# Two heads on the two halves of the TensorE array: the k-v and q products of a fused attention, MLP and gating kernel

## The chip, the cores and the metric

The kernel runs on one NeuronCore of a Trainium2 chip. The metric is the time of one execution on the device, in microseconds (us). The kernel before takes 1369.3 us, the median of 3 runs (1369.15 to 1370.15).

## The reference

Batch 8, 8 heads, sequence 576, head size 64, all float32. Three stages follow each other. The first is a linear attention with a norm over each head:

```python
kv = np.einsum('bhsd,bhse->bhde', k, v)          # per head 64 x 64
out = np.einsum('bhsd,bhde->bhse', q, kv)        # per head 576 x 64
rms = np.sqrt(np.mean(out * out, axis=-1, keepdims=True) + 1e-06)
attn = out / rms * g_norm
```

The second stage takes the result as x (8 x 576 x 512), adds a low-rank product along the sequence (u = x + (x^T U V)^T) and an MLP with 2048 hidden units (u + relu(u w_ch1) w_ch2). The third is a gated MLP: h = gelu(x w_in), its second half normalised and mixed along the sequence by w_sg (576 x 576), multiplied with the first half, then w_out and the residual. Only the first stage's two products, kv and out, are touched by the change.

## The kernel before, in words

**Stages.** In the first 60 us the attention of batch 0 is computed. Then the up products of the MLP (x w_ch1, by a scheme of seven products on blocks) run for batch 0 to 7, one tile per batch; into the steps of tile t the attention of batch t + 1 is interleaved. After some 515 us the down products follow (to about 945 us) and then the gated MLP. Large products are done as three products of a high and a low part (`product`, L1366 to L1368).

**Attention.** Two heads make a pair; HP = 4 pairs a batch, 32 in all. k_raw, v_raw and q_raw hold a pair's inputs, rows on the partitions in NJ = 5 groups (the last of 64 rows, padded with zeros). For one pair m:
- `q_transposed` (transposes at L1371) puts q of both heads, 64 + 64 columns, on the partitions: qT is 128 x 5 x 128, the first head on partitions 0 to 63, the second on 64 to 127. ScalarE copies it out of PSUM (`q_copy` L656, `q_copy_tail` L660).
- `k_v` (L1387) multiplies k^T and v of both heads at once: 5 accumulating products of 128 x 128 by 128 x 128. Only the two 64 x 64 blocks on the diagonal are wanted. `kv_copy` (L666 on ScalarE in the loop, L1067 on VectorE in the first rounds) copies these two into kv, whose other two blocks were set to zero once, by a memset on GpSimd (POOL, L594).
- `attention` (L1395, L1397) multiplies qT (stationary, 128 x 128 for each of the 5 groups) with the block-diagonal kv (moving, 128 x 128). Four groups fill one PSUM bank (BX = 6), the fifth goes to the next (BY = 7).
- ScalarE copies the result into y, in two activations (`attn_copy`, L671 for the bank of four groups, L673 for the fifth), then squares it (L677). VectorE sums the squares (L968), ScalarE takes the root (L681), VectorE inverts and multiplies (L972, L975), then high and low parts are made (L685, L979), and `low_rank` (L1403) and `u_transposed` (L1371, L1414) finish the pair. The result leaves by x_raw (L697).

All these products are plain float32. Each appears in the trace as two passes, and a pass is one LDWEIGHTS (engine row PEld) and one MATMUL (engine row PE). So the 5 products of k_v or of attention are 10 passes.

**What orders the work.** Each engine's program is written out by hand, and semaphores tie them. In the up stage a tile has STEPS = 56 steps of 6 products. `attention_step` hangs the pair's pieces behind certain steps of a period of 12: attention behind step 0, q_transposed and k_v of the next pair behind step QK = 2, low_rank behind step 8, u_transposed behind step 11. Before q_transposed PE waits for s_o, the counter of y copies, since the transposes go into the banks that attention filled. Before attention it waits for s_uev, the copy of the former pair's result. s_out counts finished parts of attention, s_zero the memsets at the start. VectorE's sums of the up products (`added`, L1047 to L1061) free the PSUM banks for PE's next steps.

Of the kernel before, what the change touches and what calls it, by code (L numbers as in the profile page):

```python
# [7 lines left out]
ACT = mybir.ActivationFunctionType  # L8
AX = mybir.AxisListType

P = 128
B, H, S, HD = 8, 8, 576, 64
# [5 lines left out]
NJ = 5  # L18
JM = 4
# [6 lines left out]
HP = H // 2  # L26
# [53 lines left out]
def build(nc, q, k, v, g_norm, U, V, w_ch1, w_ch2, w_in, g_ln, w_sg, b_sg, w_out, out):  # L80
# [35 lines left out]
    k_raw = at("k_raw", [P, NJ, 2, HD], F32)  # L116
    v_raw = at("v_raw", [P, 2, NJ, HD], F32)
    q_raw = at("q_raw", [P, NJ, 2, HD], F32)
    qT = at("qT", [P, NJ, P], F32)
    part = at("part", [P, P], F32)  # L120
    kv = at("kv", [P, P], F32)
    y = at("y", [P, NJ, P], F32)
# [19 lines left out]
    k_raw = [k_raw] + [at(f"k_raw{i}", [P, NJ, 2, HD], F32) for i in range(1, HP)]  # L142
# [71 lines left out]
    with ExitStack() as ctx:  # L214
# [7 lines left out]
        s_zero = sem("tails_zeroed")  # L222
# [357 lines left out]
        @block.gpsimd  # L580
        def _(pool):

            nc.gpsimd.memset(identF[:], 0.0).then_inc(s_zero, 1)
            for i in range(HP):
                nc.gpsimd.memset(k_raw[i][:, JM, :, :], 0.0).then_inc(s_zero, 1)
                nc.gpsimd.memset(v_raw[i][:, :, JM, :], 0.0).then_inc(s_zero, 1)
                nc.gpsimd.memset(q_raw[i][:, JM, :, :], 0.0).then_inc(s_zero, 1)
            nc.gpsimd.memset(eps_col[:], EPS).then_inc(s_zero, 1)
            nc.gpsimd.memset(half_neg[:], -0.5).then_inc(s_zero, 1)
            nc.gpsimd.memset(U_raw[:, JM, :], 0.0).then_inc(s_zero, 1)  # L590
            pool.wait_ge(s_zero, 3 * HP + 4)
            nc.gpsimd.affine_select(out=identF[:], in_=identF[:], compare_op=ALU.not_equal, fill=1.0, base=0,
                                    pattern=[[-1, P]], channel_multiplier=1).then_inc(s_idF, 1)
            nc.gpsimd.memset(kv[:], 0.0).then_inc(s_zero, 1)  # L594
            nc.gpsimd.memset(V_aug[:, S:].bitcast(F32), 0.0).then_inc(s_zero, 1)
            pool.dma_start(U_raw[:, 0:JM, :], U[0:SM, :].rearrange("(p j) r -> p j r", j=JM)).then_inc(s_small, 16)
            pool.dma_start(U_raw[0:ST, JM, :], U[SM:S, :]).then_inc(s_small, 16)
            for n in range(4):
                pool.dma_start(V_raw[R * n:R * (n + 1), :], V[:, :]).then_inc(s_small, 16)

            def load_w1(part, pairs):

                for slot, kh, fh in ((0, 0, 0), (4, 0, 1), (3, 1, 0), (6, 1, 1)):
                    for c in range(2):
                        at_ = slice(0, 2) if part == 0 else slice(pairs.start - 2, pairs.stop - 2)
                        pool.dma_start(w1_raw[min(part, 1)][:, at_, 1, slot, c * P:(c + 1) * P],
                                       w_ch1[(2 * kh + c) * P:(2 * kh + c + 1) * P,
                                             (NPAIR * fh + pairs.start) * P:(NPAIR * fh + pairs.stop) * P].rearrange("p (a m) -> p a m", m=P)
                                       ).then_inc(s_w1[part], 16)

            pool.wait_ge(s_kv, 1)
            load_w1(0, slice(0, 2))
            pool.wait_ge(s_kv, 3)
            load_w1(1, slice(2, 4))
            pool.wait_ge(s_kv, HP)
            load_w1(2, slice(4, NPAIR))
            for g in range(2, NG):
                pool.wait_ge(s_p, 2 * NI * (g - 2) + 4)
                w1_sums(pool, nc.gpsimd, g)


            def x2_low(p, par):
                n = (NJ * P, S)[par]
                pool.wait_ge(s_x2hi, 2 * p + par + 1)
                nc.gpsimd.tensor_tensor(x2_lo[par][:, :, 0:n], x2_raw[par][:, :, 0:n], x2_hi[par][:, :, 0:n].bitcast(F32),
                                        ALU.subtract).then_inc(s_x2lo, 1)

            def inverse_std(p, par):
                for j in range(VB[par], VB[par + 1]):
                    pool.wait_ge(s_var, NCP * p + j + 1)  # L630
                    nc.gpsimd.tensor_tensor(rs[:, j % 3, :], ve[:, j % 3, :], half_neg[:], ALU.pow).then_inc(s_rs, 1)

            pool.wait_ge(s_pb, NSL * (NTILE - 1) + 24)
            nc.gpsimd.memset(ws_raw[:, 0:JM, SM:SM + ST], 0.0).then_inc(s_wst, 1)
            nc.gpsimd.memset(ws_raw[:, 0:JM, SM + 2 * ST:], 0.0).then_inc(s_wst, 1)
            nc.gpsimd.memset(ws_raw[:, JM, :], 0.0).then_inc(s_wst, 1)
            inverse_std(0, 0)
            x2_low(0, 1)
            with pool.Fori(0, B // 2 - 1) as i:
                inverse_std(i, 1)  # L640
                x2_low(i + 1, 0)
                inverse_std(i + 1, 0)
                x2_low(i + 1, 1)
            inverse_std(B // 2 - 1, 1)
# [3 lines left out]
        def _(act):  # L648
            def bank(n, a, b):
                return ps[:, n, a:b]  # L650

            def q_copy(m, bx, first=False):
                act.wait_ge(s_qt, 2 * m + 1)
                if not first:
                    act.wait_ge(s_out, 2 * m)
                nc.scalar.activation(qT[:, 0:JM, :].rearrange("p j m -> p (j m)"), ps[:, bx], ACT.Copy).then_inc(s_qsb, 1)  # L656

            def q_copy_tail(m, by):
# [8 lines left out]

            def attn_copy(m, bx, by, y=y):

                act.wait_ge(s_out, 2 * m + 1)  # L670
                nc.scalar.activation(y[:, 0:JM, :].rearrange("p j m -> p (j m)"), ps[:, bx], ACT.Copy).then_inc(s_o, 1)  # L671
                act.wait_ge(s_out, 2 * m + 2)
                nc.scalar.activation(y[:, JM, :], bank(by, 0, P), ACT.Copy).then_inc(s_o, 1)  # L673

            def squares(m, sq, y=y):
                act.wait_ge(s_o, 2 * (m + 1))
                nc.scalar.activation(sq[:], y[:], ACT.Square).then_inc(s_sq, 1)  # L677

            def std(m):
# [54 lines left out]
            for n in range(2):  # L734
                act.dma_start(gcol[HD * n:HD * (n + 1), :], g_norm.rearrange("(p o) -> p o", o=1)).then_inc(s_g, 16)

            act.wait_ge(s_zero, 3 * HP + 6)
            q_copy(0, 0, first=True)
            q_copy_tail(0, 1)
            for m in range(HP):  # L740
# [224 lines left out]
        def _(dve):  # L965
# [100 lines left out]
                    o = slice(HD * n, HD * (n + 1))  # L1066
                    nc.vector.tensor_copy(kv[o, o], ps[o, bx, o]).then_inc(s_kvsb, 1)  # L1067

            dve.wait_ge(s_zero, 3 * HP + 6)
            kv_copy(0, 2)  # L1070
            low_rank_factors()
            for m in range(HP):
# [288 lines left out]
        def _(pe):  # L1361
# [19 lines left out]
            def k_v(m, bx, slot, times, at_=0):  # L1381

                pe.wait_ge(s_k[slot], 48 * times)
                pe.wait_ge(s_v[slot], 32 * times)
                n = slot if isinstance(m, int) and m < HP else 0
                for j in range(NJ):
                    ins = mm(ps[:, bx, at_:at_ + P], k_raw[n][:, j], v_raw[n][:, :, j, :], start=(j == 0), stop=(j == NJ - 1))  # L1387
                ins.then_inc(s_kv, 1)

            def attention(m, bx, by):  # L1390

                pe.wait_ge(s_kvsb, 2 * (m + 1))
                pe.wait_ge(s_qsb, 2 * (m + 1))
                for j in range(JM):
                    ins = mm(ps[:, bx, j * P:(j + 1) * P], qT[:, j], kv[:], start=True, stop=True)  # L1395
                ins.then_inc(s_out, 1)
                mm(ps[:, by, 0:P], qT[:, JM], kv[:], start=True, stop=True).then_inc(s_out, 1)  # L1397

            def low_rank(m, bn_):

# [24 lines left out]
            q_k_v_first(0)  # L1425
            for m in range(HP):
                if m:
                    pe.wait_ge(s_o, 2 * m)
                attention(m, BX, BY)
                if m > 1:  # L1430
                    u_transposed(m - 2, 4, y_first[m - 2])
                q_k_v_first(m + 1)
                if m == 1:
                    pe.wait_ge(s_low, 3)
                if m:
                    low_rank(m - 1, 3)
# [7 lines left out]
            def attention_step(k, t, end):  # L1444

                r, at_ = hook(k)
                m = HP * (t + 1) + r
                more = r + 1 < HP or not end
                if at_ == 0:
                    pe.wait_ge(s_uev, m)  # L1450
                    attention(m, BX, BY)
                elif at_ == QK and more:
                    pe.wait_ge(s_o, 2 * (m + 1))
                    q_transposed(m + 1, BX, BY, (r + 1) % HP, t + 2 + (r + 1) // HP)
                    k_v(m + 1, BY, (r + 1) % HP, t + 2 + (r + 1) // HP, P)
                elif at_ == LOW:
                    if more:
                        pe.wait_ge(s_qsb, 2 * (m + 1) + 1)
                    low_rank(m, BX)
                elif at_ == UT:  # L1460
                    if more:
                        pe.wait_ge(s_qsb, 2 * (m + 2))
                        pe.wait_ge(s_kvsb, 2 * (m + 2))
                    u_transposed(m, BX)
# [198 lines left out]
```

## Time and profile before

| | us |
|---|---|
| median of 3 runs | 1369.3 |
| the profiled execution | 1368.81 |
| its span, first to last instruction | 1367.0 |
| PE busy with matmuls | 1307.4 |
| VectorE busy | 868.1 |
| ScalarE busy | 541.6 |
| POOL busy | 97.9 |

The profile comes from one execution. In it PE stands for matmuls and PEld for the weight loads, which run beside them; DVE is VectorE, ACT ScalarE, POOL GpSimd, SP SyncE. A matmul's length is modelled and overlaps with the next one's start; the distance between two starts is what one really takes. The mean TensorE clock granted was 0.992 of full speed. "L1387" is a line of the kernel; lines of helpers are shared, and the names beside them (ps<-kv,qT) tell which product it is.

### The profile page before, as it was taken

What the parts mean: (1) busy time and instruction counts of PE and PEld (TensorE: products, weight loads), DVE (VectorE), ACT (ScalarE), POOL (GpSimd) and SP (SyncE); (2) the same over time, 40 slices, a digit from 0 to 9 for tenths busy, and PEclk for the clock granted to TensorE, in tenths of its full rate; (3) what the DMA queues carried; (4) which work ended last, traced back from release to release, by engine and by line L of the source; (5) the groups of instructions that cost most, each with busy time, mean ns of one, the idle gap of its engine ahead of it and who ended that gap; (6) DMA issues with size and microseconds to landing.
All of it is one profiled execution on the core that took longest, in us unless ns stands there. A gap on an engine that the chain in (4) does not pass through costs nothing.

```text
span 1367.0 us, 22208 instructions
## 1 busy us (share of the span) xinstructions
PE 1307.4 (96%) x8590; PEld 1254.3 (92%) x8590; DVE 868.1 (64%) x1228; ACT 541.6 (40%) x892; POOL 97.9 (7%) x107
## 2 busy tenths in 40 slices
PE   5799999999999998999999999999999999999998
PEld 5688999999999988989999999998898998998987
DVE  4977575656565758888888888885642624425322
ACT  4554434444343432455444454535222322223221
POOL 6220000000000000000000000000210210111100
PEclk9999999999999999999999999999999999999999
DMA  9444445454545426736537174441012021120211
GB/s 233 126 139 130 148 132 155 131 165 149 163 131 158 131 96 217 274 124 221 173 104 257 55 271 146 162 154 60 19 60 79 10 77 39 49 77 23 66 39 39
DMA packets 182023, 170.27 MB, mean 125 GB/s; under 512 B 94112, under 2 KB 152496, under 8 KB 181952
## 3 DMA queue, kind: packets, MB, share of 16 engines
q1 hardware_dynamic: 178992, 164.42, 38.1%
q0 software_dynamic: 1600, 4.56, 1.2%
q8 instruction: 50, 0.82, 0.2%
q10 hardware_dynamic: 1360, 0.30, 0.1%
q14 instruction: 21, 0.17, 0.0%
HBM read 101.08 MB, written 66.06 MB: 122 GB/s over the span
## 4 chain that ended last, share of the span: by engine, by line
PE 83%; DVE 8%; ACT 3%; issue 2%; DMA 2%; SPq 1%; POOL 0%; DVEq 0%; ACTq 0%; POOLq 0%
PE ps L1366 24%; PE ps L1368 24%; PE ps L1367 24%; PE ps L1371 3%; PE ps L1395 2%; PE ps L1387 2%; PE ps L1403 1%; DVE w L1008 1%; DMA hT_scratch<-h_st 1%; DVE x_lo L1035 1%; DVE h_st L1059 1%; PE ps L1614 1%; PE ps L1615 1%; DVE y L975 1%; ACT w L702 1%
## 5 line engine op out<-in xcount | busy, mean ns | idle before, releaser
L1366 PE MATMUL ps<-x_hi,w 128*128 128x288 f32 x896 | 273.6, 305 | 26.4 <-DVE h_st L1059 7.5
L1367 PE MATMUL ps<-x_lo,w 128*128 128x288 f32 x896 | 266.3, 297 | 0.0
L1368 PE MATMUL ps<-x_hi,w 128*128 128x288 f32 x896 | 265.9, 297 | 0.0
L1366 PE MATMUL ps<-r_hi,w_hi 128*128 128x384 f32 x672 | 225.0, 335 | 3.0 <-DVE r_lo L1187 1.9
L1368 PE MATMUL ps<-r_hi,w_lo 128*128 128x384 f32 x672 | 224.5, 334 | 0.0
L1367 PE MATMUL ps<-r_lo,w_hi 128*128 128x384 f32 x672 | 224.5, 334 | 0.0
L827 ACT ACTIVATE r_hi<-hb 128x768 fp32r<-128x768 f32 x168 | 142.2, 848 | 169.3 <-PE ps L1368 164.3
L1366 PEld LDWEIGHTS ps<-x_hi,w 128*128 128x128 f32 x896 | 170.1, 190 | 31.8 <-DVE h_st L1061 7.9
L1367 PEld LDWEIGHTS ps<-x_lo,w 128*128 128x128 f32 x896 | 170.5, 190 | 0.0
L1368 PEld LDWEIGHTS ps<-x_hi,w 128*128 128x128 f32 x896 | 170.5, 190 | 0.0
L1329 DVE SCALAR_TENSOR_TENSOR vs<-ps,glcol,bias_bc 128x576 f32<-128x576 f32 x32 | 26.1, 815 | 199.8 <-PE ps L1615 199.5
L1187 DVE TENSOR_TENSOR r_lo<-hb,r_hi 128x768 fp32r<-128x768 f32 x120 | 114.4, 956 | 33.7 <-ACT r_hi L827 33.7
L1366 PEld LDWEIGHTS ps<-r_hi,w_hi 128*128 128x128 f32 x672 | 126.1, 188 | 4.5 <-issue 2.5
L1368 PEld LDWEIGHTS ps<-r_hi,w_lo 128*128 128x128 f32 x672 | 126.1, 188 | 0.0
L1367 PEld LDWEIGHTS ps<-r_lo,w_hi 128*128 128x128 f32 x672 | 126.1, 188 | 0.0
L1366 PE MATMUL ps<-ws_hi,vn_hi 128*128 128x288 f32 x256 | 75.7, 296 | 0.0
L1366 PE MATMUL ps<-x_hi,wu_hi 128*128 128x288 f32 x256 | 75.6, 295 | 0.0
L1368 PE MATMUL ps<-x_hi,wu_lo 128*128 128x288 f32 x256 | 75.5, 295 | 0.0
L1367 PE MATMUL ps<-ws_lo,vn_hi 128*128 128x288 f32 x256 | 75.4, 294 | 0.0
L1368 PE MATMUL ps<-ws_hi,vn_lo 128*128 128x288 f32 x256 | 75.4, 294 | 0.0
L1367 PE MATMUL ps<-x_lo,wu_hi 128*128 128x288 f32 x256 | 75.4, 294 | 0.0
L1366 PE MATMUL ps<-wo_hi,ga_hi 128*128 128x512 f32 x144 | 60.2, 418 | 0.6 <-DVE ga_lo L1319 0.6
(166 smaller groups left out, 2494.9 us busy)
## 6 DMA issues: line engine op xcount, KB each, us to landing
hT_scratch<-h_st SPq DMA_DIRECT2D x64, 576.0 KB, 4.7
hb<-hT_scratch SPq DMA_DIRECT2D x24, 1536.0 KB, 7.2
uT_scratch<-x_raw SPq DMA_DIRECT2D x32, 288.0 KB, 2.3
x_st<-uT_scratch SPq DMA_DIRECT2D x24, 384.0 KB, 3.5
x2T_scratch<-x_st SPq DMA_DIRECT2D x24, 384.0 KB, 6.8
x_raw<-x2T_scratch SPq DMA_DIRECT2D x8, 1152.0 KB, 6.0
k_raw<-in_k SPq DMA_DIRECT2D x64, 128.0 KB, 3.0
v_raw<-in_v SPq DMA_DIRECT2D x32, 256.0 KB, 3.0
```

Source lines behind the costliest of these rows:

```text
L702: nc.scalar.activation(w1[a // 2][:, a % 2, 0], w1_raw[min(a // 2, 1)][:, a if a < 2 else a - 2, 1], ACT.Copy).then_inc(s_w1hi, 1)
L827: nc.scalar.activation(r_hi[:, n % RING], piece(h_source(i), q_), ACT.Relu if i in (3, 6) else ACT.Copy).then_inc(s_hhi, 1)
L975: nc.vector.tensor_tensor(yv, yv, rstd[:].unsqueeze(2).to_broadcast([P, 2 * NJ, HD]), ALU.mult).then_inc(s_y, 1)
L1008: nc.vector.tensor_tensor(w1[a // 2][:, a % 2, 1], w1_raw[min(a // 2, 1)][:, a if a < 2 else a - 2, 1], w1[a // 2][:, a % 2, 0].bitcast(F3 ...
L1187: ins = nc.vector.tensor_tensor(lo, x, hi, ALU.subtract)
L1329: nc.vector.scalar_tensor_tensor(vs[:, c % 2, :].rearrange("p (a m) -> p a m", a=2), us_tile(c), glcol[:, c:c + 1], bias_bc[:].rearrange(" ...
L1366: mm(dst, ws[0], xs[0], start=first, stop=False)
L1367: mm(dst, ws[0], xs[1], start=False, stop=False)
L1368: return mm(dst, ws[1], xs[0], start=False, stop=last)
L1371: return mm(dst, src, identF[:], is_transpose=True, start=start, stop=stop)
L1387: ins = mm(ps[:, bx, at_:at_ + P], k_raw[n][:, j], v_raw[n][:, :, j, :], start=(j == 0), stop=(j == NJ - 1))
L1395: ins = mm(ps[:, bx, j * P:(j + 1) * P], qT[:, j], kv[:], start=True, stop=True)
```

## The change

k_v does each head by itself. For each of the 5 groups there are two products: k of one head (128 rows, 64 columns) stationary on one column half of the array, and v of the same head (64 columns) moving. The output of the first head goes to partitions 0 to 63 of the bank, that of the second to 64 to 127, in the places where the diagonal blocks were.

attention does each head by itself too. For each group and head, qT of the head (64 partitions, 128 columns) is stationary on one row half of the array, and the head's 64 x 64 block of kv is moving. The first head writes bank BX, the second bank BY, 5 x 64 columns in each.

The memset of kv is left out, and the y copy is one activation that reads both banks. The counters s_out and s_o go up by one for a pair instead of two, and the waits on them and on s_zero are changed to match.

```diff
-            nc.gpsimd.memset(kv[:], 0.0).then_inc(s_zero, 1)
...
             def attn_copy(m, bx, by, y=y):
 
-                act.wait_ge(s_out, 2 * m + 1)
-                nc.scalar.activation(y[:, 0:JM, :].rearrange("p j m -> p (j m)"), ps[:, bx], ACT.Copy).then_inc(s_o, 1)
-                act.wait_ge(s_out, 2 * m + 2)
-                nc.scalar.activation(y[:, JM, :], bank(by, 0, P), ACT.Copy).then_inc(s_o, 1)
+                act.wait_ge(s_out, m + 1)
+                nc.scalar.activation(y[:].rearrange("p j (h d) -> p h j d", h=2),
+                                     ps[:, bx:by + 1, 0:NJ * HD].rearrange("p h (j d) -> p h j d", j=NJ), ACT.Copy).then_inc(s_o, 1)
...
                 for j in range(NJ):
-                    ins = mm(ps[:, bx, at_:at_ + P], k_raw[n][:, j], v_raw[n][:, :, j, :], start=(j == 0), stop=(j == NJ - 1))
+                    for h in range(2):
+                        o = slice(HD * h, HD * (h + 1))
+                        ins = mm(ps[o, bx, at_ + HD * h:at_ + HD * (h + 1)], k_raw[n][:, j, h], v_raw[n][:, h, j, :],
+                                 start=(j == 0), stop=(j == NJ - 1), tile_position=(0, HD * h))
                 ins.then_inc(s_kv, 1)
...
-                for j in range(JM):
-                    ins = mm(ps[:, bx, j * P:(j + 1) * P], qT[:, j], kv[:], start=True, stop=True)
+                for j in range(NJ):
+                    for h in range(2):
+                        o = slice(HD * h, HD * (h + 1))
+                        ins = mm(ps[:, (bx, by)[h], j * HD:(j + 1) * HD], qT[o, j], kv[o, o], start=True, stop=True, tile_position=(HD * h, 0))
                 ins.then_inc(s_out, 1)
-                mm(ps[:, by, 0:P], qT[:, JM], kv[:], start=True, stop=True).then_inc(s_out, 1)
```

## Rows read from the trace of the kernel before

**Rows 1.** The page, busy time of each engine and its share of the span.
```profile
PE 1307.4 (96%) x8590; PEld 1254.3 (92%) x8590; DVE 868.1 (64%) x1228; ACT 541.6 (40%) x892; POOL 97.9 (7%) x107
```

**Rows 2.** Windows: length; PE, PEld, DVE, ACT, POOL busy (instructions); clock, DMA share, GB/s.
```profile
0.00:60.00 60.00, 36.50 (x236) 34.15 (x236) 40.58 (x73) 32.78 (x61) 28.51 (x56) 0.94 0.82 199
60.00:515.00 455.00, 434.57 (x3313) 425.36 (x3313) 293.16 (x468) 191.07 (x403) 10.64 (x6) 0.99 0.46 139
```

**Rows 3.** Groups of PE instructions, 125 to 515 us: busy us, mean ns, idle before.
```profile
L1387 PE MATMUL ps<-v_raw,k_raw 128*128 128x128 f32 x230 | 29.4, 275 | 0.0
L1395 PE MATMUL ps<-kv,qT 128*128 128x128 f32 x192 | 27.2, 284 | 0.6
...
L1397 PE MATMUL ps<-kv,qT 128*128 128x128 f32 x48 | 9.3, 275 | 0.0
```

**Rows 4.** Waits of PE, 125 to 515 us: total us, times, longest.
```profile
PE ps L1366 <- DVE h_st L1061: 6.6, 7, 1.4
PE ps L1366 <- DVE h_st L1059: 6.2, 7, 1.3
```

**Rows 5.** Chain of waits, 300 to 345 us: start, us held, by what.
```profile
320.17 0.89 PE ps L1395 x8
321.06 0.22 PE ps L1397 x2
...
322.88 0.55 PE ps L1371 x5
323.42 1.12 PE ps L1387 x10
```

**Rows 6.** Timeline, 81.4 to 81.9 us: start, us, engine, what; transposes after a wait.
```profile
81.43 0.20 PEld L1371 LDWEIGHTS ps<-identF,y 128*128 128x128 f32 x2 [2.45 <-issue]
81.46 0.41 PE L1371 MATMUL ps<-identF,y 128*128 128x128 f32 x2 [2.24 <-DVE a_aug L988]
81.60 0.19 PEld L1414 LDWEIGHTS ps<-V_aug,a_aug 128*128 128x128 f32 x1
...
81.73 0.24 PEld L1371 LDWEIGHTS ps<-identF,y 128*128 128x128 f32 x2
```

**Rows 7.** Timeline of the weight loads, 319.0 to 319.6 us: up products after a wait.
```profile
319.10 0.19 PEld L1366 LDWEIGHTS ps<-x_hi,w 128*128 128x128 f32 x1 [1.09 <-DVE h_st L1059]
319.21 0.19 PEld L1367 LDWEIGHTS ps<-x_lo,w 128*128 128x128 f32 x1
```

**Rows 8.** Groups of ScalarE's instructions, 125 to 515 us: the squares of y.
```profile
L677 ACT ACTIVATE sq<-y 128x640 f32<-128x640 f32 x24 | 17.8, 742 | 0.8
```

**Rows 9.** Timeline, 200 to 240 us: from attention to low_rank of one pair.
```profile
205.04 0.39 PE L1397 MATMUL ps<-kv,qT 128*128 128x128 f32 x2
...
205.24 0.60 ACT L671 ACTIVATE y<-ps 128x512 f32<-128x512 f32 x1 [1.25 <-PE ps L1395]
...
205.73 0.27 ACT L673 ACTIVATE y<-ps 128x128 f32<-128x128 f32 x1
...
206.85 0.71 PE L1371 MATMUL ps<-identF,q_raw 128*128 128x128 f32 x5
...
210.81 0.82 DVE L979 TENSOR_TENSOR y_hl<-y,y_hl 128x640 fp32r<-128x640 f32 x1 [1.63 <-ACT y_hl L685]
...
213.30 0.76 PE L1403 MATMUL ps<-y_hl,U_aug 128*128 128x256 f32 x5
```

**Rows 10.** Chain of waits, 0 to 60 us: attention and y of the first pair.
```profile
14.04 2.06 PE ps L1395 x8
16.12 0.60 ACT y L671
```

**Rows 11.** Timeline, 0 to 60 us: the memset of kv, and the first k-v product.
```profile
3.32 0.20 POOL L594 MEMSET kv<- 128x128 f32 x1
...
8.43 2.47 PE L1387 MATMUL ps<-v_raw,k_raw 128*128 128x128 f32 x10 [8.43 <-DMA v_raw<-in_v]
```

**Rows 12.** Timeline of VectorE, 299.9 to 319.3 us: what PE's wait hangs on.
```profile
306.18 0.75 DVE L1061 TENSOR_TENSOR h_st<-ps,h_st 128x576 f32<-128x576 f32 x1
```

More of the change, by code:

```diff
@@ L654, in q_copy @@
                 if not first:
-                    act.wait_ge(s_out, 2 * m)
+                    act.wait_ge(s_out, m)
                 nc.scalar.activation(qT[:, 0:JM, :].rearrange("p j m -> p (j m)"), ps[:, bx], ACT.Copy).then_inc(s_qsb, 1)
@@ L668, in attn_copy @@
             def attn_copy(m, bx, by, y=y):
-                act.wait_ge(s_out, 2 * m + 1)
-                nc.scalar.activation(y[:, 0:JM, :].rearrange("p j m -> p (j m)"), ps[:, bx], ACT.Copy).then_inc(s_o, 1)
-                act.wait_ge(s_out, 2 * m + 2)
-                nc.scalar.activation(y[:, JM, :], bank(by, 0, P), ACT.Copy).then_inc(s_o, 1)
+                act.wait_ge(s_out, m + 1)
+                nc.scalar.activation(y[:].rearrange("p j (h d) -> p h j d", h=2),
+                                     ps[:, bx:by + 1, 0:NJ * HD].rearrange("p h (j d) -> p h j d", j=NJ), ACT.Copy).then_inc(s_o, 1)
             def squares(m, sq, y=y):
-                act.wait_ge(s_o, 2 * (m + 1))
+                act.wait_ge(s_o, m + 1)
                 nc.scalar.activation(sq[:], y[:], ACT.Square).then_inc(s_sq, 1)
@@ L735, in _ @@
                 act.dma_start(gcol[HD * n:HD * (n + 1), :], g_norm.rearrange("(p o) -> p o", o=1)).then_inc(s_g, 16)
-            act.wait_ge(s_zero, 3 * HP + 6)
+            act.wait_ge(s_zero, 3 * HP + 5)
             q_copy(0, 0, first=True)
@@ L1067, in kv_copy @@
                     nc.vector.tensor_copy(kv[o, o], ps[o, bx, o]).then_inc(s_kvsb, 1)
-            dve.wait_ge(s_zero, 3 * HP + 6)
+            dve.wait_ge(s_zero, 3 * HP + 5)
             kv_copy(0, 2)
@@ L1427, in _ @@
                 if m:
-                    pe.wait_ge(s_o, 2 * m)
+                    pe.wait_ge(s_o, m)
                 attention(m, BX, BY)
@@ L1452, in attention_step @@
                 elif at_ == QK and more:
-                    pe.wait_ge(s_o, 2 * (m + 1))
+                    pe.wait_ge(s_o, m + 1)
                     q_transposed(m + 1, BX, BY, (r + 1) % HP, t + 2 + (r + 1) // HP)
```

## The prediction

> **What bounds the kernel now.** I began with the page's busy times: TensorE is busy for 96% of the span, the next engine for 64% [rows 1]. The table by stage then says where a change of these products can count: all of them lie in the first 60 us (4 of the 32 head pairs) and in the stage from 60 to 515 us (28 pairs), where PE is busy 434.57 of 455 us and VectorE 293 [rows 2]. The groups of instructions of the steady part show what PE does there: mostly the up products, and beside them the products to be changed, 230 passes of k-v and 192 + 48 passes of q-kv [rows 3]. Each float32 product is two passes of a weight load and a matmul: 5 products, 10 passes, and 230 is 23 rounds, 240 is 24. The list of waits has PE idle only twice in a tile of about 65 us, 1.3 to 1.4 us each time, both for VectorE's sums [rows 4]. The chain of waits runs through PE in every round, so what a round's products take stands in the time one for one: k-v holds the chain for 1.12 us, q-kv for 0.89 + 0.22 us: 10 passes at 0.11 us, the pitch in both [rows 5].
>
> **What sets the pitch of a pass.** This decides the case, since the change makes 20 passes of 10, each with half of the columns to stream. Three rows bear on it. First, the matmul: the full-width transposes have the same 128 columns of float32 and go at 0.11 us (five in 0.55 us of the chain [rows 5]), although their weight loads follow each other after only 0.06 us (two loads of 0.14 us each fill 0.20 us [rows 6]). So 128 columns of float32 stream in about 0.107 us, and 64 in about 0.054. Second, the load: where PE starts after a wait, the second load begins 0.11 us after the first [rows 7], with nothing in front of it but the first load. So an ordinary load of 128 columns takes about 0.11 us, as long as today's matmul; in the present products the two lie beside each other and both fill the pitch. Third, issue: in the transposes load, matmul and second load begin at 81.43, 81.46 and 81.49 (0.20 less 0.14) [rows 6]; no row shows a pair in less than 0.06 us.
> The Trainium skill ("TensorE: Matmul & The Clock Gate", LDWEIGHTS) gives a load's time as its columns divided by 1.2 GHz, whatever the rows in use; for 128 columns that is 107 ns, and the trace agrees with 0.11 us.
>
> **The change part by part**, per head pair, against 1.12 us for each product set:
> - *q-kv on row halves.* Ten products, 20 passes. The stationary side is qT of one head: 64 partitions, but still 128 columns. The moving side is kv, 64 columns. Bounds: from 0.56 us (two heads truly side by side, half of 1.12) to 2.2 us (20 loads of 0.11 in a row). I take 2.2: the matmul is halved, but the load is the longer of the two and each pass has its own. +1.08 us, times 32 = +34.6 us.
> - *k-v on column halves.* 20 passes, 64 columns stationary and 64 moving. Bounds: 0.56 us, and 2.2 us if a load has a fixed time. I take 0.06 a pass, the pitch of issue and also half of the present stream with its few ns of overhead: 1.20 us, +0.08, times 32 = +2.6 us.
> - *Changing the array's shape.* The up products and transposes stay on the full array, so each round goes full, row halves, full, column halves, full: 4 changes. No row shows one. Bounds: nothing, since the trace's change from a product back to transposes costs 0.02 us over a load (81.60 to 81.73 [rows 6]); and 0.27 us, when the last matmul has to end first (0.27 us long at a pitch of 0.11, so 0.16 are left) and then a load stands bare (0.11). I take the bare load, 0.11, as the nearest: 0.44 a round, times 32 = +14 us.
> - *More instructions.* 20 loads and 20 matmuls more in a round are in the pitches above. SP, POOL and DMA issue nothing new and no DMA is moved; the loads of q, k and v that wait on SP for a round's products start as much later as PE is, and are used a round later.
> - *One y copy for two.* ScalarE has 0.60 + 0.27 us today [rows 9], and 0.742 for a pass over the same 640 elements (the squares) [rows 8], which I take for the new copy: about 0.13 less work on an engine that waits for PE anyway. But it can only start after the last pass, where the first copy today starts after the eighth of ten (205.24 [rows 9]). Today the copies end at 206.00, 0.57 us after the last matmul's end at 205.43; the new one ends about 0.78 after. PE needs y at the transposes of q, 206.85 [rows 9], so 0.85 us of cover become 0.65: nothing. The squares, the sum and the normalised y come 0.2 us later; low rank begins at 213.30 and y_low ended at 211.63 [rows 9], so that is covered too, with 1.6 us. In the first four rounds nothing covers it, since there the chain goes from q-kv straight to y [rows 10]: 4 x 0.2 = +0.8 us. The first of these rounds has its eight passes in 2.06 us [rows 10] where the steady ones have 0.89 [rows 5]; I price all rounds at the steady pitch, which could be 1 to 2 us too little.
> - *The memset of kv is gone.* 0.2 us of POOL at 3.3 us [rows 11], while PE waits for v until 8.43 [rows 11]: nothing. The waits on the zeroing counter only get earlier. Were the load of v earlier than 4 us, it would be worth at most that 0.2.
> - *What is hidden.* One of PE's two waits in a tile hangs on the end of VectorE's chain behind a k-v step (the sum of L1061 [rows 4], here from 306.18 to 306.93 [rows 12], five us after k-v); what k-v and its two changes of shape add there, 0.3 us, comes out of that wait: 7 tiles, -2.1 us. What q-kv adds is hidden by nothing, since VectorE's sums wait for PE and move along with it.
> Sum: 34.6 + 2.6 + 14 + 0.8 - 2.1 = **+50 us**. The profiled execution took 1368.8 us (span 1367.0 and 1.8 around it), 0.5 under the median of 1369.3; **1368.8 + 50 = 1419 us**.
>
> **A rule that speaks against the change, beside mine.** The rows show no change of shape, so its price above is a choice. The Trainium skill ("TensorEngine Tiling (Array Packing)", Tiling Modes) says that a change of tiling mode drains TensorE. By that rule each change would be at the upper bound of 0.27 us, the term 35 us in place of 14, and the sum +71 (1440 us); that is the upper part of the forecast's case, some 0.15 of its 0.50, and no row here bears it out or speaks against it.
>
> **Rivals.**
> 1. *The load shrinks too* (or the loads of the two row halves overlap), and issue sets every pass at 0.06 us: q-kv +2.6 us like k-v, with the changes of shape 2.6 + 2.6 + 14 + 0.8 - 2.1 = +18, so 1387 us; 1373 with free changes. For it: only half of the rows are loaded. Against: in the trace the load is a matter of its own 0.11 us and not of the matmul beside it.
> 2. *The two heads really run side by side*: load and matmul of one half beside those of the other. Each product set takes 0.56 us. Gain 2 x 0.56 x 32 = 36 us; the changes of shape give back 14, and the covered wait grows by 0.56 - 0.22 in each of 7 tiles, 2 us: -20, so **1349 us**, 1335 with free changes. It decides as soon as the mean pitch of the 40 passes falls under (2.24 - 0.44)/40 = 0.045 us, or 0.056 if the changes are free. For it: the heads use different rows or columns, and q-kv different banks. Against: no pair in the trace goes faster than 0.06, and both passes of one product stand one behind the other on the same half.
>    The Trainium skill ("TensorE: Matmul & The Clock Gate", Packing small matmuls) states that matmuls on different tiles of the array start about 4 ns apart and gives 3.07 times the speed for four row tiles; by that rule this rival is what happens, though its cases stream 512 columns behind each load, which no row here does with a tile.
> 3. *Nothing to measure*: the pitch halves exactly and no change of shape costs anything: 20 x 0.056 = 1.12, 1369 us.
>
> **How the numbers follow.** Forecast (load-bound q-kv, 1404 with free changes of shape to 1472 with full drains and k-v load-bound as well) 0.50; rival 1, 0.20; rival 2, 0.25; rival 3, 0.05. Rival 2 is kept this high because nothing in the trace uses half of the array. The range: the forecast's upper end counts little, since it needs both dear bounds at once, so 1450 leaves out some 0.07; at the low end 1348 takes in half of rival 2, leaving out some 0.12. About 0.2% (2.7 us) is what a measurement of this kernel tells from no change. Faster 0.25, within it 0.06, slower 0.69. The forecast's own range is 1400 to 1450.
>
> **What would show it.** In the profile after: 20 loads and 20 matmuls a round on each of the two product lines. Right, if the loads of q-kv follow each other at 0.11 us and those of k-v at 0.06, and if a gap of about 0.11 us stands before the first pass after each change. Rival 1 shows as 0.06 in both; rival 2 as matmuls of the two halves that start almost together, with a step of 0.03 or less on average, and as a longer wait of PE for VectorE in each tile. The y copy should be one activation of about 0.74 us, with no wait of PE for it outside the first rounds. The forecast is wrong if q-kv takes under 1.5 us a round, or if the stage from 60 to 515 us grows by less than 28 x 1.1 = 31 us.

## The result and the profile after

The change takes 1373.1 us (median of 12 runs, 1371.4 to 1376.9) against 1369.2 for the kernel before (1366.7 to 1370.2): 1.0034 times as long, 95% interval 1.0025 to 1.0043. A second series gave 1.0032 (1.0020 to 1.0044). So it is slower, as forecast, but by 4 to 5 us and not by 50. All ratios here are of fast executions; of the twelve of one kernel below (the change with filler), two took 2131 and 3276 us and are not in its ratio.

The profiled execution has a span of 1375.1 us and is the longest of its twelve. The page and the table by stage of the kernel after, which answer to [rows 1, 2]; the line numbers of most PE work are two lower or a few higher than before (up products L1364 to L1366, transposes L1369, q-kv L1398):

```profile
PE 1316.0 (96%) x9230; PEld 1251.6 (91%) x9230; DVE 866.6 (63%) x1228; ACT 539.7 (39%) x860; POOL 96.5 (7%) x106
```
```profile
0.00:60.00 60.00, 41.99 (x352) 38.08 (x353) 38.74 (x73) 33.00 (x56) 26.88 (x55) 0.86 0.80 195
60.00:515.00 455.00, 432.36 (x3798) 414.11 (x3797) 286.63 (x457) 186.23 (x371) 10.86 (x6) 0.98 0.45 139
```

There are 640 passes more on PE, as said (32 rounds x 20), and the granted clock (the first figure behind the engines) is lower in both stages: 0.86 and 0.98, where it was 0.94 and 0.99.

The groups of PE, VectorE's hold on PE and ScalarE's y copy, 125 to 515 us, which answer to [rows 3, 4, 8]:

```profile
L1398 PE MATMUL ps<-kv,qT 64*128 64x64 f32 x480 | 32.4, 278 | 1.7 <-issue 1.1
...
L1387 PE MATMUL ps<-v_raw,k_raw 128*64 128x64 f32 x460 | 19.0, 231 | 0.0
```
```profile
PE ps L1364 <- DVE h_st L1057: 6.5, 7, 1.7
PE ps L1364 <- DVE h_st L1059: 6.5, 6, 1.4
PE ps L1398 <- issue: 1.1, 1, 1.1
```
```profile
L670 ACT ACTIVATE y<-ps 128x640 f32<-128x640 f32 x24 | 16.9, 704 | 30.8 <-PE ps L1398 30.8
```

Twice the passes, yet k-v keeps PE busy for 19.0 us where it was 29.4 [rows 3], and q-kv for 32.4 where it was 27.2 + 9.3. The two waits for VectorE are there as before, and a new one stands in the last line: once, for 1.1 us, PE stood in the middle of a q-kv set (the 20 passes of one pair of heads), and no semaphore explains it. The y copy is one activation of 0.70 us.

How the passes lie, from the timeline: the first loads and matmuls of a q-kv set, then the first two matmuls of a k-v set; and the chain of waits through the same round, to be held against [rows 5]:

```profile
206.25 0.30 PEld L1398 LDWEIGHTS ps<-kv,qT 64*128 64x128 f32 x4 [0.27 <-ACT x_raw L695]
206.26 0.44 PE L1398 MATMUL ps<-kv,qT 64*128 64x64 f32 x4
```
```profile
209.85 0.28 PE L1387 MATMUL ps<-v_raw,k_raw 128*64 128x64 f32 x2
```
```profile
206.26 1.33 PE ps L1398 x20
207.59 0.33 PE ps L1364
...
209.38 0.55 PE ps L1369 x5
209.92 0.73 PE ps L1387 x20
210.66 0.33 PE ps L1364
```

Two matmuls of 0.27 us fill 0.28 us, so the second head's starts 0.01 us after the first's (6 ns by the trace's start times). Four loads of 0.19 us fill 0.30: two start together, the next two 0.11 later. The halves work side by side, loads and all. Twenty passes of k-v hold the chain for 0.73 us instead of 1.12; twenty of q-kv hold it for 1.33, where ten held it for 1.11. And behind each set the next up matmul holds it for 0.33 instead of 0.14: the change back to the full array.

Added up over one steady tile (four rounds, all distances between starts of matmuls on PE), in us:

| a steady tile of the up stage | before | after | difference |
|---|---|---|---|
| within the q-kv sets | 4.32 | 4.24 | -0.08 |
| from up to q-kv | 1.11 | 1.20 | +0.09 |
| from q-kv to up | 0.12 | 0.81 | +0.69 |
| within the k-v sets | 4.02 | 2.32 | -1.70 |
| from the transposes of q to k-v | 0.44 | 0.81 | +0.37 |
| from k-v to up | 0.12 | 0.61 | +0.49 |
| between up matmuls, with the waits | 45.70 | 45.89 | +0.19 |
| whole tile | 64.82 | 64.86 | +0.04 |

The rest is equal to 0.01, the two waits for VectorE too: 2.55 us a tile in both kernels. The 0.19 stands behind the first up matmul after each set (0.10 after k-v, 0.09 after q-kv), so I count it with the changes of shape. In the steady rounds, then, the change gains 0.45 us a round and pays 0.46 for four changes of shape: nothing is left. The four are not alike: up to q-kv costs 0.02 us, transposes to k-v 0.09, k-v to up 0.12 and q-kv to up 0.17, and the last two 0.02 more each behind the first up matmul. The loss of 4 us is elsewhere.

### The profile page after: what moved, and what is told of

Same layout as the page of the kernel before. It is cut to its first block, busy times and chain, and to the rows that moved or that the text cites. A ratio compares the mean times of both kernels' runs of the same rounds, so it can differ in the third digit from the quotient of the medians.

```text
span 1375.1 us, 23435 instructions
## 1 busy us (share of the span) xinstructions
PE 1316.0 (96%) x9230; PEld 1251.6 (91%) x9230; DVE 866.6 (63%) x1228; ACT 539.7 (39%) x860; POOL 96.5 (7%) x106
## 4 chain that ended last, share of the span: by engine, by line
PE 86%; DVE 7%; ACT 3%; issue 2%; DMA 1%; POOL 0%; SPq 0%; DVEq 0%; ACTq 0%; POOLq 0%
PE ps L1364 25%; PE ps L1366 24%; PE ps L1365 24%; PE ps L1369 4%; PE ps L1398 3%; PE ps L1387 2%; PE ps L1405 1%; DVE w L1006 1%; DVE h_st L1057 1%; PE ps L1616 1%; PE ps L1617 1%; PE ps L1416 1%; ACT w L700 1%; DVE w_lo L1157 0%; DMA wc_raw<-in_moe_w_out 0%
## 5 line engine op out<-in xcount | busy, mean ns | idle before, releaser
L1364 PE MATMUL ps<-x_hi,w 128*128 128x288 f32 x896 | 276.6, 309 | 27.3 <-DVE h_st L1057 8.3
L1366 PE MATMUL ps<-x_hi,w 128*128 128x288 f32 x896 | 267.6, 299 | 0.0
L1364 PE MATMUL ps<-r_hi,w_hi 128*128 128x384 f32 x672 | 225.2, 335 | 3.7 <-DVE r_lo L1185 2.6
L1366 PE MATMUL ps<-r_hi,w_lo 128*128 128x384 f32 x672 | 224.7, 334 | 0.0
L1364 PEld LDWEIGHTS ps<-x_hi,w 128*128 128x128 f32 x896 | 171.4, 191 | 36.6 <-DVE h_st L1059 7.9
L1366 PEld LDWEIGHTS ps<-x_hi,w 128*128 128x128 f32 x896 | 172.0, 192 | 0.0
L1364 PEld LDWEIGHTS ps<-r_hi,w_hi 128*128 128x128 f32 x672 | 126.2, 188 | 5.2 <-issue 3.1
L1366 PEld LDWEIGHTS ps<-r_hi,w_lo 128*128 128x128 f32 x672 | 126.2, 188 | 0.0
L1364 PE MATMUL ps<-ws_hi,vn_hi 128*128 128x288 f32 x256 | 75.7, 296 | 0.0
L1364 PE MATMUL ps<-x_hi,wu_hi 128*128 128x288 f32 x256 | 75.6, 295 | 0.0
L1366 PE MATMUL ps<-x_hi,wu_lo 128*128 128x288 f32 x256 | 75.5, 295 | 0.0
L1366 PE MATMUL ps<-ws_hi,vn_lo 128*128 128x288 f32 x256 | 75.5, 295 | 0.0
L1364 PE MATMUL ps<-wo_hi,ga_hi 128*128 128x512 f32 x144 | 60.2, 418 | 0.6 <-DVE ga_lo L1317 0.6
```

Of the source, the lines that this page charges most:

```text
L1364: mm(dst, ws[0], xs[0], start=first, stop=False)
L1366: return mm(dst, ws[1], xs[0], start=False, stop=last)
```

## The experiments

All times stand beside runs of the kernel before on the same chip; ratios are to these.

**The parts apart.** Only k-v on halves (the new k_v in the kernel before):

> Only the k-v products are on column halves; q-kv, its two y copies and the memset are as before. In the profile of the changed kernel a round's transposes and k-v product take 1.50 us instead of 1.71, so this part by itself gains 0.21 us a round. Theory A (k-v gains, q-kv on halves loses 0.12 us a round): 28 x 0.21 = 5.9 us of PE's work is gone, less what VectorE's waits take back, so faster than before by 3 to 6 us, about 1365. Theory B (what is lost is lost in the clock, since products on halves let TensorE fall to half clock more often): slower than before or equal in spite of the shorter rounds, 1369 to 1373, with more time at half clock than the kernel before has.

1362.7 us, ratio 0.9961 (0.9948 to 0.9974). Only q-kv on halves (the change with the old k_v):

> Only q-kv is on row halves, with the one y copy and no memset; the k-v products are as before. Theory A: 28 x 0.12 = +3.4 us, and some more in the first four rounds, so about 1373 to 1374, as slow as the whole change. Theory B: the same sign, but the steady tiles of the up stage (64.8 us each in both profiles) are unchanged or 0.5 us longer each, and the rest of the loss stands beside stretches at half clock.

1374.4 us, ratio 1.0045 (1.0030 to 1.0059). A tile runs from the first q-kv matmul of one to that of the next; the timeline of the kernel before, of k-v alone, of q-kv alone and of the change, each with the starts of the same two tiles:

```profile
320.00 0.27 PE L1395 MATMUL ps<-kv,qT 128*128 128x128 f32 x1
...
384.82 0.27 PE L1395 MATMUL ps<-kv,qT 128*128 128x128 f32 x1
```
```profile
316.48 0.39 PE L1398 MATMUL ps<-kv,qT 128*128 128x128 f32 x2
...
380.56 0.38 PE L1398 MATMUL ps<-kv,qT 128*128 128x128 f32 x2
```
```profile
319.51 0.33 PE L1395 MATMUL ps<-kv,qT 64*128 64x64 f32 x2
...
385.12 0.33 PE L1395 MATMUL ps<-kv,qT 64*128 64x64 f32 x2
```
```profile
326.74 0.33 PE L1398 MATMUL ps<-kv,qT 64*128 64x64 f32 x2
...
391.59 0.33 PE L1398 MATMUL ps<-kv,qT 64*128 64x64 f32 x2
```

64.82, 64.08, 65.61 and 64.85 us. The parts are -0.74 and +0.79 a tile, -5.2 and +5.5 us over 7 tiles: that is what the two kernels measured against the one before (-5.3 and +6.2, by the ratios). So theory A's account holds for each part alone, with q-kv dearer than it said (0.20 us a round and not 0.12). Together they make nothing, in the sum and in the change's own tile. The change is almost 4 us slower than the sum of its parts (+4.6 against +0.9).

**The y copy alone.** The kernel before with

```diff
-   four groups: y[:, 0:JM] <- ps[:, bx]; then the fifth: y[:, JM] <- ps[:, by, 0:P]
+   y[:] <- 640 columns from the start of bank bx, once attention is done
```

> The kernel before with one y copy in place of two (it reads 640 columns of the two banks in one piece) and nothing else. Prediction's step: nothing in the steady rounds, +0.2 us in each of the first four, so 1369 to 1371. Rival: the later start of the copy is seen in the waits, 0.2 us a round, 1375.

1367.0 us, 0.9988 (0.9979 to 0.9996). The later start costs nothing that shows. The small gain may be the clock's: these runs had a mean clock of 0.9935, those of before 0.9918. With k-v on halves beside it:

> k-v on column halves, q-kv on the full array with its memset, one y copy of 640 columns in one piece, no filler. If the two gains add (0.9961 and 0.9988 of the kernel before, measured): 0.995, 1361.5 us. Rival: the y copy's gain was its runs' luck with the clock (18 us at half clock against 22.5), and the time is that of k-v on halves alone, 1363.

1365.0 us, 0.9974 (0.9962 to 0.9985), where k-v alone had 0.9961 (0.9948 to 0.9974): no gain was added. That the one copy is worth anything is not shown.

**What sets the pitch of q-kv on halves.** In the change,

```diff
-   ps[:, (bx, by)[h], j * HD:(j + 1) * HD], qT[o, j], kv[o, o]
+   ps[:, (bx, by)[h], j * HD:(j + 2) * HD], qT[o, j], kv[o, o] read twice (64 + 64 columns)
```

> The changed kernel with 128 moving columns instead of 64 in each q-kv product (the 64 columns of kv are read twice, and the next group overwrites the second copy). If the weight load sets the pitch of q-kv on halves (0.112 us for two passes side by side, the load of 128 columns being 0.108), the pitch stays at 0.112 and the time at 1373 to 1374 us. If the matmul or the issue of instructions set it, twice the columns make it 0.16 us or more, +0.5 us a round, 1389 us.

1374.9 us. The chain of this kernel, then of the change, a q-kv set of the same round:

```profile
339.60 1.39 PE ps L1398 x20
```
```profile
340.76 1.33 PE ps L1398 x20
```

Twice the columns cost 0.06 us a set and not 0.5, and 0.05 of it stands between the first two pairs of passes; the pairs behind follow at 0.112 us in both. So the stream does not set the pitch. k-v has loads of 64 columns and streams the same 64: its pair of passes takes 0.058 us. What is left for q-kv is its load of 128 columns, which half of the rows makes no shorter. (Row halves with a load of 64 columns were not run, so that row halves as such are slower is not shut out by a run.) A first form of this kernel, with a wider tile for kv, gave no result.

**How far apart the heads may stand.** In the change's k_v the loops are exchanged:

```diff
-   for j in range(NJ): for h in range(2):
+   for h in range(2): for j in range(NJ):
```

> The changed kernel, but in each k-v product set the five products of the first head stand ahead of the five of the second. In the change the two heads alternate and their passes start 6 ns apart, ten pairs in 0.58 us. If a pass of the second head can only run beside the first's where it stands near it in the program (within a few instructions), the set takes 20 x 0.058 = 1.16 us, +0.58 us a round, 1373 + 17 = 1390 us. If each half of the array takes its instructions from the queue by itself (10 loads and 10 matmuls ahead is within its depth), nothing changes: 1373.

1384.0 us, 1.0109 (1.0094 to 1.0123), between the two forecasts. The chain of one round, and the windows of one k-v set (in the brackets the matmuls and the loads that lie in the window or reach into it):

```profile
346.84 0.55 PE ps L1369 x5
347.38 1.13 PE ps L1387 x20
```
```profile
210.42:210.82 0.40, 0.39 (x6) 0.39 (x7) 1.00 0.00 0
210.82:211.05 0.23, 0.23 (x10) 0.23 (x9) 1.00 0.00 0
```

The set takes 1.13 us where the alternating one takes 0.73. In its first 0.40 us only one half works: 7 loads (the alternating set begins 14 in as long). Then, at 210.83 us by the trace's start times, loads and matmuls begin in pairs, two matmuls 4 to 6 ns apart, and the rate doubles: the second head has started while the first still has three matmuls to go. After three such pairs one half works alone again, to the end of the set, and so in each of 16 sets. (The records do not name the head; this is read from the starts.) So PE takes work for the idle half ahead of its turn only from close by: the second head's first load went ahead of the five instructions that were left of the first head's ten passes, and not ahead of more.

**The price of a change of shape.** k-v alone on halves, with its set cut in two around the transpositions, in the 28 rounds of the loop:

```diff
-   q_transposed (4 + 1 transposes); k_v groups 0..4
+   transpose of group 4; k_v groups 0, 1; 4 transposes; k_v groups 2..4
```

> k-v on column halves and q-kv as before (1363 us), but in the 28 rounds of the up stage the k-v set is cut in two, groups 0 and 1 behind the transposition of q's last group and groups 2 to 4 behind the transpositions of its first four: two changes of shape more in each round. By the gaps in the profile of the change (0.202 us from the last full matmul to the first on halves instead of 0.109, and 0.152 to the next full one instead of 0.031) that costs 0.21 us a round: 28 x 0.21 = +6.0, 1369 us, less what VectorE's waits hide. If those gaps are something else than the change of shape (the wait for v, the first pair's start), +0 to +2 us.

1373.0 us, 1.0027 (1.0017 to 1.0037), against 0.9961 uncut: 9 us for 56 changes of shape, where the gaps would have made 6. Its chain, from the first transpose to the last of k-v:

```profile
349.48 0.11 PE ps L1371
349.59 0.38 PE ps L1389 x8
349.97 0.58 PE ps L1371 x4
350.56 0.50 PE ps L1389 x12
```

Four transposes now hold the chain for 0.58 us where five held it for 0.55, and the two parts of k-v for 0.88 instead of 0.73. The gaps are the changes' price, then: in the change 0.11 to 0.12 us each on average (0.46 for four), in this kernel 0.15 each.
The Trainium skill ("TensorEngine Tiling (Array Packing)", Tiling Modes) says that a change of mode drains the engine; the trace agrees as far as the distance between two matmuls grows at each of the four, by 0.02 to 0.17 us. On average that is about one bare load of 128 columns, and each is under the 0.27 that the prediction worked out for a full wait for the last matmul and a load; so these traces do not show a full drain at that price.

**Where the 4 us are.** The runs' mean clock gave the lead. The twelve runs of the change have 0.9884 on average, which is 2 x 0.0116 x 1373.6 = 32 us at the lower level (1.2 GHz); those of before, in the first series of experiments, 0.9918 or 22 us. At that level PE does half as much, so up to (32 - 22)/2 = 5 us. Filler products in the waits of the first 60 us, in both kernels:

```diff
+   for _ in range(n): mm(ps[:, BX, 0:P], identF[:], identF[:], start=True, stop=True)
```

> The kernel before, with filler products of the identity with itself (128x128, result never read) in the places of the first 60 us where PE waits: 8 ahead of the first k-v product, then 4, 3, 3 and 6 ahead of the first four q-kv products, 6, 6 and 5 ahead of the last two u_transposed and of the first up step. Theory B (TensorE falls to half clock where it idles in the first rounds, and the runs' spread is that): less time at half clock than the 22.5 us that the runs of before had on average, by 10 to 17 us, and 4 to 8 us faster, about 1362. Rival (the first rounds hang on ScalarE, VectorE and DMA, the clock there costs nothing): 1368 to 1370.

> The changed kernel with the same filler. The clock records say that the changed kernel's runs spend 32 us at half clock on average against 22.5 of the kernel before, and each run's time less half of that is 1357.7 against 1357.4. Theory B: with the filler in both the two kernels come together, this one within 1.5 us of the kernel before with filler. Rival (the loss is a fixed cost of the first rounds, where the changes of shape stand bare on the path): still 3 to 5 us slower than the kernel before with filler.

1369.5 us for before with filler (1.0003, 0.9993 to 1.0012), with a mean clock of 0.9937, so 5 us less at the lower level, and nothing gained; 1368.5 for the change with filler (0.9997, 0.9987 to 1.0007), with a mean clock of 0.9921. The two kernels came together as theory B said: the filler took the whole loss of 5 us off the change. But the theory's other half failed: in the kernel before a higher clock in the first 60 us brought nothing. Either it costs little there, where PE waits for other engines, or the filler costs what it brings; these runs don't tell the two apart. Nor did the filler help the best pair:

> k-v on column halves, q-kv on the full array as before with its memset, one y copy of 640 columns in one piece, and the filler. If the parts add: -5.5 (k-v on halves, measured) and the filler's gain, 1357 to 1360, faster than every other kernel here. If the filler is worth nothing, 1362 to 1363.

1366.6 us, 0.9987 (0.9975 to 0.9998): no better than the same without filler (0.9974, 0.9962 to 0.9985), and a little worse than k-v alone (0.9961, 0.9948 to 0.9974).

The traces held against each other showed a place. The timeline of the kernel before, and of the change run once more (1373.4 us), with the starts of tiles (that of before at 320.00 stands above):

```profile
255.26 0.38 PE L1395 MATMUL ps<-kv,qT 128*128 128x128 f32 x2
```
```profile
255.49 0.35 PE L1398 MATMUL ps<-kv,qT 64*128 64x64 f32 x2
...
323.60 0.33 PE L1398 MATMUL ps<-kv,qT 64*128 64x64 f32 x2
...
388.46 0.33 PE L1398 MATMUL ps<-kv,qT 64*128 64x64 f32 x2
```

> The change itself once more, beside the others, for its clock. Theory B: again about 30 us at half clock against 22 of the kernel before, a time of 1372 to 1374, and in the profile again a fall to half clock near 255 us, where the second pass through the loop of tiles begins. Rival: the fall at 259.5 us in its one profile was chance; then none of the kind here.

At 255 us both are level (0.2 us apart; in the change's first profile it is 2.6); the next tile takes 68.11 us instead of 64.74; the one behind it 64.86 again. The chain of the change there, and the windows from 250 to 262 us (last but two: the clock) of the change again, of before, of q-kv alone and of k-v on halves with one y copy:

```profile
253.38 1.13 issue
254.51 0.39 PE ps L1364
...
255.56 1.78 PE ps L1398 x16
257.34 0.19 issue
257.53 0.69 PE ps L1398 x4
258.22 0.54 PE ps L1364
258.76 0.24 PE ps L1365
```
```profile
250.00:262.00 12.00, 9.87 (x62) 9.16 (x61) 8.63 (x15) 4.73 (x9) 0.00 (x0) 0.74 0.28 102
```
```profile
250.00:262.00 12.00, 10.72 (x85) 10.49 (x84) 10.48 (x17) 7.05 (x15) 0.00 (x0) 1.00 0.38 127
```
```profile
250.00:262.00 12.00, 10.69 (x92) 10.23 (x91) 10.11 (x16) 6.25 (x13) 0.00 (x0) 1.00 0.44 139
```
```profile
250.00:262.00 12.00, 11.24 (x100) 11.01 (x101) 8.92 (x14) 6.53 (x14) 0.00 (x0) 1.00 0.57 175
```

The clock falls to 1.2 GHz, at 255.7 us and for 6.8 us, and an up matmul takes 0.24 us instead of 0.13. Before it fell, PE had 2.2 us between the starts of two matmuls and then did six up matmuls and the first passes of q-kv. Of the 5.0 us between the spans of this profile and of before, 3.4 stand in this tile, 0.2 came before it, and 1.4 come behind it. It fell at that place in all five profiles of kernels with both sets on halves (at 255 to 260 us), 0.8 to 2.6 us after the wait's end, and in none of the eight others taken by then (the expectation below counts seven). The wait is the first return to the head of the loop of tiles: in all kernels it is longer than at the other tiles (1.5 to 2.2 us against 1.14 to 1.24), partly for VectorE and partly for nothing that the profile shows. A wait of 1.9 to 2.0 us did not bring the fall in the three kernels with q-kv on the full array, nor one of 1.6 us in the kernel with q-kv alone on halves.

The test: five filler products in that wait, at every tile's start but the first, in the change and as a control in the kernel before.

> The change with five filler products of the identity (1.1 us, result never read) at the start of each tile of the up stage but the first, where PE waits 1.1 to 2.2 us for VectorE. The steady tiles of the change take what those of before take (64.8 us), but in five profiles out of five of kernels with both sets of products on halves the clock falls to half for 6.8 us at 255 to 260 us, behind that wait and the q-kv set, and the tile takes 3 to 4 us longer; in seven profiles of other kernels it does not. Theory B1 (the fall comes from the idle time followed by a q-kv set that runs on halves): with the filler the fall is gone and the time is 3 to 4 us shorter than the change's, 1369 to 1370. Rival (the fall hangs on something else there, as the fetch of instructions at the second pass through the loop): it stays, 1373 or more.

> The kernel before with the same filler at the start of each tile: there is no fall of the clock near 255 us to be taken away, so 1368 to 1370, unless the filler outlasts the wait (some 0.1 us a tile) or costs something that would then have to be taken off the gain of its sister.

The change with filler: 1371.4 us, 1.0014 (1.0004 to 1.0024) instead of 1.0034 (1.0025 to 1.0043). The control: 1369.0 us, 1.0001 (0.9992 to 1.0010). The windows of the change with filler at the place, and the starts of the tile:

```profile
250.00:262.00 12.00, 10.49 (x86) 9.90 (x86) 9.53 (x14) 3.90 (x7) 0.00 (x0) 1.00 0.32 118
```
```profile
258.77 0.33 PE L1398 MATMUL ps<-kv,qT 64*128 64x64 f32 x2
...
324.00 0.33 PE L1398 MATMUL ps<-kv,qT 64*128 64x64 f32 x2
```

The fall is gone and the tile takes 65.23 us. With it went 2 to 3 us of the loss, 0.2% of the time: less than the 3 to 4 that were expected, and the two intervals barely part. What is left, about 2 us, is not shown to a place. It may be the first stage's: in its profile this kernel had a clock of 0.77 in the first 60 us, where before had 0.94, and its four quickest runs (1369.1 to 1369.6) have a mean clock of 0.991 to 0.994. The other filler, in the first 60 us, points there too. It took off 5 us, more than this one, and in its one profile (the longest of the ten) the fall at 254.7 us was still there; up to 130 us that profile had 13.7 us at the lower level, as before had, where the change had 27.3 and 20.5. So the two gains do not add up to the loss, and how the 5 us divide between the first stage and this tile stays open.

The theory as I worded it is only half borne out. That the wait takes part is shown by the filler. That the q-kv set behind it does, is not: with 128 columns streamed the clock fell 0.3 us before the first pass of that set, at 257.0 us. Why it fell only where both sets run on halves stays open.

## Why the prediction was wrong

**What bounds the kernel** held: PE's products stand in the time one for one, the parts' tiles differ by just what their sets take, and VectorE's chain hid nothing of q-kv.

**Load, stream and issue.** The load of 128 columns takes 0.11 us, half rows or not, and sets q-kv's pitch: this was right, and the doubled stream left the pitch as it was. The failed step is the next one: "each pass has its own", 20 loads of 0.11 in a row. Two loads run side by side, one for each half, so it is ten times 0.11: **q-kv was priced at +1.08 us a round and is -0.02**. That alone is 35 of the 50 us.

**k-v** was priced at +0.08 us a round and is -0.42: two heads side by side in pairs at 0.058 us. The floor of 0.06 us for a pair "no row shows" was no floor of issue: 20 passes start in 0.58 us. I had taken the quickest pitch of a trace that never needed a quicker one for a limit. The term was +2.6 us where it should have been -13.6.

**The changes of shape** were priced at 0.44 us a round and are 0.46. The bare load was the right bound to be near on average, the drain of 0.27 each was not; that the sum came out so well is in part luck, since singly they cost 0.02 to 0.19.

**The hidden part** was priced at -2.1 us and is nothing. PE's waits for VectorE are 2.55 us a tile before and after, so k-v's gain did not make them longer either, as rival 2 had it; and with the heads apart, where k-v takes 0.40 us more, they are still 1.32 and 1.14 to 1.24 us. **The y copy**: 0.70 us, nothing exposed. **The memset**: nothing.

By the measured sets, changes and tiles the steady rounds give 0, and rival 3 (nothing to measure) would have come nearest, but for another reason than the one it gave. Rival 2 had the mechanism, at 0.25, and with its own sizes wrong: it halved q-kv too, which the load forbids. Had I joined its first half (side by side) to my load, the sum would have been -0.02 - 0.42 + 0.44 = 0. That the change came out slower at all, as forecast, is luck: none of the forecast's terms made it so, and what was found of the loss hangs on the clock.

**What no step had**: the clock. None asked what the changed sets, with a wait, do to TensorE's level. About half of the measured loss went when the wait at 255 us was part filled, and all of it when the waits of the first 60 us were.

The Trainium skill ("TensorE: Matmul & The Clock Gate", Packing small matmuls) has matmuls on different tiles about 4 ns apart; the trace agrees, with 6 ns. It adds that loads overlap with matmuls in flight only where the row group differs; the k-v halves differ in columns alone, and yet their loads start 6 ns apart, two in the 0.058 us that one takes where one half works alone. Here the measurement goes against it.

**The better kernel.** k-v on column halves and q-kv left on the full array: 1362.7 us, 0.9961 of the kernel before and 10 us less than the change.

## What to carry to other kernels

Halves of the array work side by side, loads included, if the products alternate within about three passes. What a pair of passes then takes is the longer of load and stream: the product whose stationary side kept its 128 columns gained nothing in float32, at 64 or 128 columns of stream, and the one that halved both took 0.58 us a set from its first matmul to its last, instead of 1.0. Set against it some 0.23 us for going to halves and back, and ask of each set by itself whether it pays.

## What was not expected of the hardware

- In a stage where PE is busy 97% of the time (126.06 of 130 us from 120 to 250 us in both kernels), one wait of 1.9 to 2.2 us stood ahead of a fall to 1.2 GHz for 6.8 us, some 3 us of time, in five of five profiles with both sets on halves; with part of the wait filled it did not fall (one profile).
- Filler that took part of the lower clock out of the first 60 us of the kernel before (0.9918 to 0.9937 on average) gained nothing (1.0003); the same filler in the change gained 5 us.
- At the first return to the head of the loop PE stands for 0.4 to 1.5 us that no semaphore explains, in all kernels, and once it stood 1.1 us within a q-kv set of 20 passes. Its cause was not tested.
